# Three-stage kernel: the last batch's folds behind two hidden tiles, the odd fold a step later, tails and table wait moved

## The reference, cut to what matters

```python
def phi(x):                       # x: (4, 8, 576, 64)
    proj = einsum('bhsd,df->bhsf', x, w_phi)           # 64 -> 128
    proj = proj - max(abs(proj), axis=-1)
    return concatenate([exp(proj), exp(-proj)], -1)
kv = einsum('bhsf,bhsd->bhfd', phi(k), v); z = sum(phi(k), axis=2)
x = (phi(q) @ kv) / (phi(q) . z + 1e-6)                # -> (4, 576, 512)

mixed = real(fft(fft(x, axis=1), axis=2)); u = x + mixed
un = (u - mean(u)) / sqrt(var(u) + 1e-6)
x = u + relu(un @ w_ch1) @ w_ch2                       # 512 -> 2048 -> 512

u = x + (relu(x.T @ w_tok1) @ w_tok2).T                # over the 576 tokens, 256 hidden
out = u + relu(u @ w_ch1b) @ w_ch2b                    # 512 -> 1536 -> 512
```

## Time and profile before

| | us |
|---|---|
| median of 3 runs | 978.4 (977.28 to 979.16) |
| profiled execution | 977.36 |
| its span, first to last instruction | 975.4 |
| PE busy | 956.0 |
| DVE, ACT, POOL busy | 477.1, 320.4, 186.3 |

### The profile page before, as it was taken

How to read it: one execution, slowest core, us unless ns; L and a number is a source line. 1 busy time by engine, 2 the same in 40 slices (tenths; PEclk the granted TensorE clock), 3 DMA queues, 4 the chain that set the end, 5 groups by cost and what they waited for, 6 DMA issues and landing times.

```text
span 975.4 us, 17951 instructions
## 1 busy us (share of the span) xinstructions
PE 956.0 (98%) x7523; PEld 861.2 (88%) x7523; DVE 477.1 (49%) x954; ACT 320.4 (33%) x631; POOL 186.3 (19%) x163
## 2 busy tenths in 40 slices
PE   8989999989999999999999999999999999999998
PEld 6989898878989999999899899877999899999997
DVE  6988888861521322222313312454684644645543
ACT  6876868544311111111111212254432212212211
POOL 3654555469700000000000000036100000000000
PEclk9999999999999999999999999999999999999999
DMA  7231333335310020010010020488220020200101
GB/s 234 78 107 48 91 113 80 114 119 200 114 65 1 1 65 1 1 65 0 0 65 0 34 80 25 140 291 294 98 87 1 1 88 1 82 5 1 44 1 44
DMA packets 50031, 70.15 MB, mean 72 GB/s; under 512 B 22948, under 2 KB 23976, under 8 KB 49832
## 3 DMA queue, kind: packets, MB, share of 16 engines
q1 hardware_dynamic: 48232, 62.84, 19.8%
q10 hardware_dynamic: 1728, 6.29, 1.8%
HBM read 50.24 MB, written 18.87 MB: 71 GB/s over the span
## 4 chain that ended last, share of the span: by engine, by line
PE 75%; POOL 2%; DMA 1%; DVE 1%; ACT 0%; issue 0%; POOLq 0%; DVEq 0%; SPq 0%
PE mlp_y L1193 7%; PE mlp_y L1194 7%; PE mlp_hid L1178 7%; PE mlp_hid L1180 7%; PE mlp_hid L1179 7%; PE mlp_y L1192 7%; PE mlp_y L1633 5%; PE mlp_y L1634 5%; PE mlp_y L1635 5%; PE mlp_hid L1620 2%; PE mlp_hid L1622 2%; PE mlp_hid L1621 2%; PE mlp_turn L1622 2%; PE mlp_turn L1621 2%; PE mlp_turn L1620 2%; DMA mlp_w_raw<-in_w_mlp 1%
## 5 line engine op out<-in xcount | busy, mean ns | idle before, releaser
L1311 DVE SCALAR_TENSOR_TENSOR mlp_h_lo<-mlp_hid,mlp_h_hi 128x384 fp32r<-128x384 f32 x96 | 53.5, 557 | 253.6 <-ACT mlp_h_hi L1228 253.5
L1228 ACT ACTIVATE mlp_h_hi<-mlp_hid 128x384 fp32r<-128x384 f32 x96 | 47.2, 492 | 288.2 <-PE mlp_hid L1180 288.2
L1178 PE MATMUL mlp_hid<-mlp_ut_hi,mlp_w_hi 128*128 128x384 f32 x384 | 130.7, 340 | 0.6 <-POOL mlp_w_lo L1140 0.6
L1180 PE MATMUL mlp_hid<-mlp_ut_hi,mlp_w_lo 128*128 128x384 f32 x384 | 129.4, 337 | 0.0
L1179 PE MATMUL mlp_hid<-mlp_ut_lo,mlp_w_hi 128*128 128x384 f32 x384 | 128.8, 336 | 0.0
L1194 PE MATMUL mlp_y<-mlp_w_hi,mlp_h_lo 128*128 128x512 f32 x288 | 113.9, 396 | 0.0
L1193 PE MATMUL mlp_y<-mlp_w_lo,mlp_h_hi 128*128 128x512 f32 x288 | 113.7, 395 | 0.0
L1192 PE MATMUL mlp_y<-mlp_w_hi,mlp_h_hi 128*128 128x512 f32 x288 | 112.6, 391 | 1.1 <-DVE mlp_h_lo L1311 1.1
L1554 POOL TENSOR_TENSOR mlp_w_lo<-mlp_w_raw,mlp_w_hi 128x1024 fp32r<-128x1024 f32 x12 | 28.4, 2397 | 393.5 <-DVE tok_x_lo L2042 390.1
L1633 PE MATMUL mlp_y<-mlp_w_hi,mlp_h_hi 128*128 128x512 f32 x216 | 84.5, 391 | 1.2 <-DVE mlp_h_lo L1828 1.2
L1634 PE MATMUL mlp_y<-mlp_w_lo,mlp_h_hi 128*128 128x512 f32 x216 | 84.4, 391 | 0.0
(11 more groups left out here) (220 smaller groups left out, 2134.2 us busy)
## 6 DMA issues: line engine op xcount, KB each, us to landing
mlp_w_raw<-in_w_mlp SPq DMA_DIRECT2D x14, 512.0 KB, 4.5
mlp_w_raw<-in_w_mlp ACTq DMA_DIRECT2D x12, 512.0 KB, 7.5
v<-in_v SPq DMA_DIRECT2D x16, 320.0 KB, 3.7
qk<-in_kT SPq DMA_DIRECT2D x16, 288.0 KB, 4.3
mlp_u<-u_scratch SPq DMA_DIRECT2D x6, 768.0 KB, 4.8
qk<-in_qT SPq DMA_DIRECT2D x15, 288.0 KB, 4.4
u_scratch<-x_all SPq DMA_DIRECT2D x4, 1024.0 KB, 4.6
mlp_u<-u_scratch SPq DMA_DIRECT2D x4, 1024.0 KB, 5.6
```

The source lines that it names most:

```text
L1178: nc.tensor.matmul(out, w_hi[:, j, col], hi, start=(c == 0), stop=False)
L1180: last = nc.tensor.matmul(out, w_lo[:, nf - 1 - j, col], hi, start=False, stop=(c == DC - 1))
L1228: nc.scalar.activation(h_hi[:, j % 2, :], hid[j % 2][:, 0:BT], ACT.Relu).then_inc(h_rounded, 1)
L1311: nc.vector.scalar_tensor_tensor(out=h_lo[:, j % 2, :], in0=hid[j % 2][:, 0:BT], scalar=0.0, in1=h_hi[:, j % 2, :], op0=ALU.max, op1=ALU.s ...
```

## The change

- PE waits for the finished table (`table_split` 5) at chunk 0 of batch 0 (step 5, slot 4) and no longer at the end of step 4.
- `third_rounded` now counts each of the two folds by itself. For batches 0 to 2 the odd fold's rounding, third tile and low part move from step k % 4 = 1 (slots 1 and 2) to k % 4 = 2, slot 0: on ACT behind qexp(0) and the exp of REST, on DVE behind that slot's piece. The even third and the edge stay.
- POOL folds the first pair of the next batch one step later, with the second.
- Pairs 3, 7 and 11 have their tails on ACT too. In steps 4, 8, 12 DVE norms in slot 2 and folds in slot 3.
- Step 15: the reciprocal root goes behind sine piece 0; `pool_add` of batch 2, tile 0, goes ahead of the fold of pair 14, tile 1 behind the last fold.
- First block of the first MLP: second 0, second 1, then chunks 0 to 4. The last even fold goes behind DVE's first low part of a hidden tile, and what ACT and DVE did for the folds beside tile 0 they do beside tile 1.

```diff
-    TAIL_ON_ACT = (4, 8, 12)
+    TAIL_ON_ACT = (3, 4, 7, 8, 11, 12)
...
         if p.n - 1 in TAIL_ON_ACT:
-            pe.wait_ge(tail_done, (p.n - 1) // 4)
+            pe.wait_ge(tail_done, TAIL_ON_ACT.index(p.n - 1) + 1)
...
     def pe_over_s(pe, b, c, out_bank):
         if c == 0:
+            if b == 0:
+                pe.wait_ge(table_split, 5)
             pe.wait_ge(fold_split, 2 * b + 1)
...
-            if k == 4:
-                pe.wait_ge(table_split, 5)
...
-        for i in {("second", 0): range(3), ("second", 1): range(3, 5), ("first", 2): range(5, len(PIECES))}.get((what, j), ()):
+        for i in {("second", 1): range(5), ("first", 2): range(5, len(PIECES))}.get((what, j), ()):
...
-    def act_third(act, b):
-
-        for rows in GROUP[0:2]:
-            last = nc.scalar.copy(fold_hi[rows, :, 0, :], folds[GROUP[0], :, 0, 0:FREQ])
+    def act_third(act, b, k):
 
         for rows in GROUP[0:2]:
             last = nc.scalar.copy(fold_hi[rows, k, 0, :], folds[GROUP[0], k, 0, 0:FREQ])
+        last.then_inc(third_rounded, 1)
...
             if s == 1 and k % 4 == 1 and 5 <= k:
+                act_third(act, k // 4 - 1, 0)
+                act_edge(act, k // 4 - 1)
+            if s == 0 and k % 4 == 2 and 6 <= k:
                 act_fold(act, k // 4 - 1, 1)
-                act_third(act, k // 4 - 1)
-                act_edge(act, k // 4 - 1)
+                act_third(act, k // 4 - 1, 1)
...
-        if j == 0:
+        if j == 1:
             act_fold(act, LAST, 0)
-            act_last_third(act, 0)
+            act_third(act, LAST, 0)
             act_edge(act, LAST)
             act_fold(act, LAST, 1)
-            act_last_third(act, 1)
+            act_third(act, LAST, 1)
             mlp1["act_weights"](act, [2])
         if j == 1:
-            for i in range(3):
+            for i in range(5):
                 act_piece(act, LAST, i)
             mlp1["act_weights"](act, [3])
-            for i in range(3, 5):
-                act_piece(act, LAST, i)
...
-    def dve_last_fold(dve):
+    def dve_last_sum(dve):
...
+    def dve_last_even(dve):
...
+            if s == 0 and k % 4 == 2 and 6 <= k:
+                dve_third(dve, k // 4 - 1, 1)
+                dve_low(dve, k // 4 - 1, 1)
+            if k % 4 == 0 and 4 <= k:
+                if s == 2:
+                    dve_norm(dve, Pair(k - 1))
+                if s == 3:
+                    dve_fold(dve, Pair(k - 1))
+            elif k % 4 == 1 and 5 <= k:
                 if s == 0:
                     dve_low(dve, k // 4 - 1, 0)
                 if s == 1:
                     dve_norm(dve, Pair(k - 1))
                 if s == 2:
-                    dve_low(dve, k // 4 - 1, 1)
-                    dve_third(dve, k // 4 - 1)
+                    dve_third(dve, k // 4 - 1, 0)
                     dve_edge(dve, k // 4 - 1)
...
-            if s == 3 and k == PAIRS - 2:
+            if s == 0 and k == PAIRS - 1:
                 mlp1["early_vector"][1](dve)
-            if s == 0 and k == PAIRS - 1:
                 dve.wait_ge(proj_done, 5 * PAIRS)
                 mlp1["early_vector"][2](dve)
...
         if j == 0:
+            dve_last_even(dve)
+        if j == 1:
             dve_low(dve, LAST, 0)
-            dve_last_third(dve, 0)
+            dve_third(dve, LAST, 0)
             dve_edge(dve, LAST)
-            dve_last_third(dve, 1)
+            dve_third(dve, LAST, 1)
             dve_low(dve, LAST, 1)
...
             mlp1["gpsimd"](pool, (), 0, 2)
+            pool_add(pool, LAST - 1, 0)
...
-        for n in ready(k):
+        for n in (k - 2, k - 1) if k % 4 == 2 and 6 <= k else () if k % 4 == 1 and 5 <= k else ready(k):
             pool_fold(pool, Pair(n))
...
         pool_last_fold(pool)
+        pool_add(pool, LAST - 1, 1)
         pool.wait_ge(fold_split, 2 * B)
         mlp1["gpsimd"](pool, (), 2, 3)
-        pool_add(pool, LAST - 1, 0)
-        pool_add(pool, LAST - 1, 1)
         pool_add(pool, LAST - 1, 2)
```

More of the change, by code:

```diff
@@ L183, in front @@
     third_rounded = sem("third_rounded")
-    last_third_rounded = sem("last_third_rounded")
     third_split = sem("third_split")
@@ L551, in act_fold @@
         nc.scalar.copy(fold_hi[:, k, 1:FRONT], folds[:, k, 1:FRONT, 0:FREQ]).then_inc(fold_rounded, 1)
-    def act_third(act, b):
-        for rows in GROUP[0:2]:
-            last = nc.scalar.copy(fold_hi[rows, :, 0, :], folds[GROUP[0], :, 0, 0:FREQ])
-        last.then_inc(third_rounded, 1)
-    def act_last_third(act, k):
+    def act_third(act, b, k):
         for rows in GROUP[0:2]:
             last = nc.scalar.copy(fold_hi[rows, k, 0, :], folds[GROUP[0], k, 0, 0:FREQ])
-        last.then_inc(last_third_rounded, 1)
+        last.then_inc(third_rounded, 1)
     def act_edge(act, b):
@@ L729, in dve_sum @@
         if p.n in TAIL_ON_ACT:
-            dve.wait_ge(tail_done, b)
+            dve.wait_ge(tail_done, TAIL_ON_ACT.index(p.n) + 1)
         if b > 0:
@@ L766, in dve_low, with dve_third @@
                                 ALU.subtract).then_inc(fold_split, 1)
-    def dve_third(dve, b):
-        dve.wait_ge(third_rounded, b + 1)
-        nc.vector.tensor_tensor(fold_hi[GROUP[2], :, 0, :], folds[GROUP[0], :, 0, 0:FREQ], fold_hi[GROUP[0], :, 0, :],
+    def dve_third(dve, b, k):
+        dve.wait_ge(third_rounded, 2 * b + k + 1)
+        nc.vector.tensor_tensor(fold_hi[GROUP[2], k, 0, :], folds[GROUP[0], k, 0, 0:FREQ], fold_hi[GROUP[0], k, 0, :],
                                 ALU.subtract)
[L774 to L778, removed]
     def dve_edge(dve, b):
@@ L816, in dve_step @@
                 dve_piece(dve, b, i)
-            if k % 4 == 1 and 5 <= k:
+            if s == 0 and k % 4 == 2 and 6 <= k:
[7 more added lines that the diff above has]
+            elif k % 4 == 1 and 5 <= k:
                 if s == 0:
@@ L860, in vector @@
         dve_norm(dve, Pair(PAIRS - 1))
-        dve_last_fold(dve)
+        dve_last_sum(dve)
     def vector_beside(dve, j):
         if j == 0:
+            dve_last_even(dve)
+        if j == 1:
             dve_low(dve, LAST, 0)
-            dve_last_third(dve, 0)
+            dve_third(dve, LAST, 0)
             dve_edge(dve, LAST)
-            dve_last_third(dve, 1)
+            dve_third(dve, LAST, 1)
             dve_low(dve, LAST, 1)
```

## The result

The changed kernel is slower: 981.28 us (977.98 to 984.37, 17 runs) for 977.12 (975.23 to 979.16, 17 runs) of the kernel before. The ratio is 1.0045, 95% interval 1.0034 to 1.0055; I had forecast no difference. The profiled execution took 983.2 us, its span 981.4.

What follows compares the result with a forecast made beforehand. The prediction took TensorE (PE), busy 956.0 of 975.4 us, as the bound. Its terms, -2.4 - 0.7 + 4.2 + 2.1 - 3.2, summed to 0.0 us, so it forecast 978.4 us, range 974.7 to 981.6.

Steps and rivals of the forecast that it cites:

- part 4: Moved odd fold, steps 6, 10, 14: PE newly waits 2.1 us at chunk 3 in each, +6.3 in all.
- Part 1: Steps 4 and 5: PE's 2.2 us wait for the table goes, some waits come back; sum -2.4 us.
- Part 2: Tails on ACT, steps 4, 8, 12: new 0.5 us wait before num, net +0.1 at steps 9 and 13.
- Part 3: Steps 9 and 13: less work before chunk 0, DVE's third shift late next; -0.35 us each, -0.7 together.
- rival E: POOL's SBUF reads meet the odd low parts in steps 6, 10, 14: 981 to 982 us, chance 0.1.
- Part 5: Steps 14 and 15: DVE late, PE waits for `ab_lo` and `ut_lo`, moved root gains nothing; +2.1 us for both.
- Part 6: First MLP's entrance: first to fourth hidden tile in 21.4 us instead of 24.6, -3.2 us.
- Rival D: Entrance keeps its wait at chunk 2 through ACT's queue; price 1.5 to 3 us, 980.9 us, chance 0.17.
- Everything after runs as before: Behind the fourth hidden tile: no change, 0 us, since POOL reaches each later weight no later than it did.

Runs made afterwards that it cites:

- after_again: The changed kernel, unaltered, timed and profiled once more: 981.73 us, ratio 1.0046 to the kernel before.
- e2: The kernel before with only the odd fold moved to step k % 4 = 2, as in the change: 983.49 us, ratio 1.0076.
- e3: The changed kernel with nine unused matmuls on PE ahead of chunk 3's wait in steps 6, 10 and 14: 979.09 us, ratio 1.0027.
- e7: The kernel before with only the first MLP's new entrance order and POOL's earlier adds of batch 2: 975.72 us, ratio 0.9985.
- e10: The kernel before with only the odd fold moved, ACT's share at the head of slot 0 in steps 6, 10, 14: 978.33 us, ratio 1.0013.
- e6: The kernel before with only the table's wait moved to chunk 0 of batch 0: 975.07 us, ratio 0.9979.
- e9: e5 with the reciprocal root back at its old place in step 14: 972.35 us, ratio 0.9949 to the kernel before.
- e11: The kernel before with unused matmuls ahead of its waits for the table (10) and for `more` (8): 975.15 us, ratio 0.9984.
- e5: e4 with the tails of pairs 3, 7, 11 back on DVE: 972.16 us, ratio 0.9948 to the kernel before.
- e1: The changed kernel with the odd fold back in its old slots, POOL's folds with it: 975.41 us, ratio 0.9991 to the kernel before.
- e4: The changed kernel with ACT's odd fold at the head of slot 0 in steps 6, 10, 14: 972.89 us, ratio 0.996 to the kernel before.
- e8: e5 with POOL's adds of batch 2 later, behind the last fold and behind the third weight: 972.28 us, ratio 0.9947.

## Why the prediction was wrong

**The step that failed is part 4's price of the new wait, 2.1 us in each of steps 6, 10 and 14.** The wait itself was right, in place, releaser and size (2.08 us from start to start). But I priced a wait of PE at its idle time alone. TensorE's clock fell behind it in two of the three steps and cost 1.6 us each time: +3.2 in this profile. The runs say the same: 16 of the 17 had a mean granted clock below 1.0, with medians of 983.2 us at 0.995 (3 runs), 982.3 at 0.997 (7), 980.2 at 0.998 (6) and 977.98 at 1.0 (1). A fall of 3.4 us at half clock lowers the mean over 981 us by 0.0017, so these are about three falls, two, one and none. As an estimate for three waits: over the profiles of after, after_again and e2 there are nine such waits and five falls, so 1.7 falls in three waits, times 1.6 is 2.7 us; e3, without falls, measured 2.2 to 2.6 less, 1.8 to 1.9 by the ratios. The two long waits in before, 2.21 and 1.73, show no fall in its profile, so I had no row against it; similar ones fell in other profiles, behind the table's wait in e7 and e10 and behind that for `more` in e6 and e9.

The Trainium skill, TensorE: Matmul & The Clock Gate, Part 1, has it that the clock is granted by how busy the engine has been just before. e3 and e11 agree with it: with the waits filled, the granted clock is 1.00 behind them. I hadn't weighed it for waits as short as these.

**Part 1, -2.4: right**, -2.54 here and -2.3 in e6.

**Part 2, +0.5 per tail: right.** 0.47 ahead of num at 60.34, three times 0.5 in the list of waits. e5 shows that the tails on DVE cost about as much, at the head of the next step.

**Part 3, -0.35 in steps 9 and 13: right in 9** (-0.42), **wrong in 13** (+0.15). DVE's third and edge, which take 0.42 us and 0.49 (step 9 of before), took 0.51 and 0.87 in step 9 and twice their time in step 13:

```profile
172.85 0.85 DVE L767 TENSOR_TENSOR fold_hi<-fold,fold_hi 32x258 fp32r<-32x258 f32 x1
173.71 0.86 DVE L774 SCALAR_TENSOR_TENSOR fold_hi<-fold_hi,mlp_ident,fold 2x258 fp32r<-2x258 f32 x1
```

POOL was adding into x in both steps, since its fold of the next batch's first pair no longer stands ahead of the adds. From num to num step 13 is 0.57 us longer than step 9. Of these, 0.25 lie in chunk 0, which waits for the edge. The other 0.32 lie in the projections before it: one shift of DVE (169.76) started 0.37 late behind its own reduction, which no run explains. I had looked for such a meeting at the odd low part in steps 6, 10 and 14 (rival E), where it didn't come about (0.69, 0.70 and 0.69 us), and not at the operations of step 13.

**Part 5, +2.1: right**, +2.25. Both waits are there, 0.95 for `ab_lo` and 1.16 for `ut_lo`, and no fall followed the wait of step 14. e9 agrees that the root's move gains nothing that can be measured.

**Part 6, -3.2: mis-sized.** Num of 15 to the fourth tile gave -2.53. First to fourth tile took 22.08 us for 21.4: two hidden tiles 4.92 for 4.6 (POOL's add in front of its fold took 3.6 us, not 3.0) and the five chunks 5.61 for 5.35. Rival D had put its wait at chunk 2; the idle there fell from 1.79 to 0.46, so D did not hold.

**"Everything after runs as before": wrong by 0.8 us.** At 265.74 PE waits 0.79 for a low part, in every profile with the new order of POOL's adds (after, after_again, e1, e3, e4, e5, e7, e9) and in none without it (before, e2, e6, e8, e10, e11). DVE and POOL in after:

```profile
253.10 11.81 POOL L1138 TENSOR_TENSOR mlp_w_lo<-mlp_w_raw,mlp_w_hi 128x1024 fp32r<-128x1024 f32 x5
...
258.48 6.47 DVE L1247 TENSOR_SCALAR mlp_var_eps<-mlp_mean_var 128x2 f32<-128x2 f32 x1
...
265.13 0.55 DVE L1309 SCALAR_TENSOR_TENSOR mlp_h_lo<-mlp_hid,mlp_h_hi 128x384 fp32r<-128x384 f32 x1
```

An operation on 2 elements per partition, whose shortest in before took 0.17, lasts 6.47 us here, to the end of five weight parts that POOL works off without a gap (264.91); the low part that PE waits for is behind it in DVE's queue. In before POOL's row of them started 0.4 us earlier relative to PE, stopped after four for want of a rounded weight, and the same operation was through in 3.61, again at the end of POOL's row (257.01 and 256.99). All eight profiles with the wait have 6.46 or 6.47 us. I had written that POOL reaches each weight no later; it was 0.4 late.

The Trainium skill, SBUF — State Buffer, section Who interferes with whom, has it that a `tensor_scalar` of DVE can take the ports that it shares with GpSimd, and that whichever of the two starts first holds them for one whole instruction while the other blocks. The trace agrees that the operation ends with POOL's work, but the time here spans more than two of POOL's instructions (2.36 us each).

**The sum.** Beside the clock: -0.14 (part 1), 0 (the idles of steps 6 and 10), +0.43 (part 3), +0.15 (part 5), +0.67 (part 6), +0.79 (the late wait) is +1.9. With 2.2 to 2.6 for the clock, by e3, this gives 4.1 to 4.5 (3.7 to 3.8 with e3's ratio); the medians differ by 4.16. That fit is in part luck: the median of before contains falls of its own, behind the two long waits that the change removes. e11, without them, is 1.1 us faster. The net cost of the clock is then smaller by up to 1.1 us, and as much of the 4.16 isn't accounted for. Between profiles the stretch from 610 to 700 us alone varies more than these terms: PE is busy between 87.3 and 89.8 of its 90 us there. In after_again all behind the fourth hidden tile took 751.5 us, +0.2 for the +0.8 of the table, though the late wait is there. So the small terms are read from their own places, and not from the span.

## What to carry to other kernels

A wait of about 2 us on an otherwise full TensorE isn't priced at its idle time: add the chance of a fall of the clock behind it times what a fall costs (here 5 in 9, times 1.6 us), and look at the scatter of the runs and at their mean granted clock, since one profile may show none. If the wait can't be moved, work that nobody needs in front of it is worth trying. Before moving a piece a step later, look at what stands ahead of it in its engine's queue: three lines moved to the head of the same slot turned +4.2 us into -3.7. On the kernel before alone the same order gained nothing (e10), so such a move has to be timed in the kernel it is meant for.

## What was not expected of the hardware

- The clock fell behind single idles of 1.7 to 2.2 us, and also behind shorter ones close together: 1.16 and 0.61 us at 9 us in after, 1.17 and 1.31 near 682 us in e6. Each of the falls read finely stood at half for 3.4 us. Behind the same wait it fell in one execution and not in the next. What decides that isn't shown.
- Filling two waits took the scatter of the runs from 4.2 to 0.8 us.
- A DVE operation of 0.17 us lasted 6.47 us, to the end of a gapless row of POOL operations, and others, of 0.42 and 0.49 us, doubled to 0.85 and 0.86 beside POOL's adds of 0.72 to 0.90 us.
